# Linear attention, Fourier mixing and two MLPs on one core: the feature projection with each head in its own 64 rows of the array, other banks, folds on GpSimd, other orders at the edges of the MLPs

## The reference

```python
def phi(x):                                   # 128 features, both signs: 256
    proj = einsum('bhsd,df->bhsf', x, w_phi)
    proj = proj - max(abs(proj), axis=-1)
    return concatenate([exp(proj), exp(-proj)])
kv = einsum('bhsf,bhsd->bhfd', phi(k), v);  z = sum(phi(k), axis=2)
x = phi(q) @ kv / (phi(q) @ z + 1e-6)         # attention, heads side by side
u = x + real(fft(fft(x, axis=1), axis=2))     # Fourier mixing
x = u + relu(normalise(u) @ w_ch1) @ w_ch2    # first MLP, 2048 hidden
u = x + (relu(x.T @ w_tok1) @ w_tok2).T       # token MLP, 256 hidden
out = u + relu(u @ w_ch1) @ w_ch2             # second MLP, 1536 hidden
```

## Time and profile before

| | |
|---|---|
| time, median of 3 runs | 996.82 us (995.91 to 997.04) |
| the profiled execution | 994.59 us |
| its span in the trace | 992.8 us |
| TensorE busy | 976.1 us |
| VectorE busy | 379.6 us |
| ScalarE busy | 285.4 us |
| GpSimd busy | 183.5 us |
| TensorE's granted clock | 1.00 of full speed throughout |

### The profile page before, as it was taken

How to read it: one execution, slowest core, us unless ns; L and a number is a source line. 1 busy time by engine, 2 the same in 40 slices (tenths; PEclk the granted TensorE clock), 3 DMA queues, 4 the chain that set the end, 5 groups by cost and what they waited for, 6 DMA issues and landing times.

```text
span 992.8 us, 17316 instructions
## 1 busy us (share of the span) xinstructions
PE 976.1 (98%) x7275; PEld 878.1 (88%) x7275; DVE 379.6 (38%) x756; ACT 285.4 (29%) x573; POOL 183.5 (18%) x161
## 2 busy tenths in 40 slices
PE   8999999999999999999999999999999999999998
PEld 6999999888899999899999999777999999999997
DVE  6998888851422222313213213553121212121211
ACT  6865656533411111111111112343111111111110
POOL 3653556279500000000000000136000000000000
PEclk9999999999999999999999999999999999999999
DMA  7242241426210010010100300775010201001000
GB/s 230 81 109 61 68 135 42 165 96 198 90 64 1 1 64 1 11 53 0 63 0 0 112 1 1 251 279 196 1 64 1 64 1 48 16 32 32 31 1 32
DMA packets 48398, 66.88 MB, mean 67 GB/s; under 512 B 22864, under 2 KB 23888, under 8 KB 48208
## 3 DMA queue, kind: packets, MB, share of 16 engines
q1 hardware_dynamic: 46608, 59.69, 18.5%
q10 hardware_dynamic: 1728, 6.29, 1.7%
HBM read 47.10 MB, written 18.87 MB: 66 GB/s over the span
## 4 chain that ended last, share of the span: by engine, by line
PE 90%; DVE 5%; POOL 2%; ACT 1%; issue 1%; DMA 1%; SPq 0%; DVEq 0%; ACTq 0%; POOLq 0%
PE mlp_y L1060 12%; PE mlp_y L1061 12%; PE mlp_hid L1045 11%; PE mlp_hid L1047 11%; PE mlp_hid L1046 11%; PE mlp_y L1059 11%; PE kv L325 3%; PE num L339 2%; PE proj L296 2%; PE mlp_turn_in L1030 1%; DVE pm L633 1%; DVE absmax L625 1%; PE proj L298 1%; PE proj L297 1%; PE four L350 1%; PE tok_y L1361 1%
## 5 line engine op out<-in xcount | busy, mean ns | idle before, releaser
L1178 DVE SCALAR_TENSOR_TENSOR mlp_h_lo<-mlp_hid,mlp_h_hi 128x384 fp32r<-128x384 f32 x168 | 93.6, 558 | 465.7 <-ACT mlp_h_hi L1095 465.6
L1045 PE MATMUL mlp_hid<-mlp_ut_hi,mlp_w_hi 128*128 128x384 f32 x672 | 229.0, 341 | 0.7 <-POOL mlp_w_lo L1007 0.7
L1095 ACT ACTIVATE mlp_h_hi<-mlp_hid 128x384 fp32r<-128x384 f32 x168 | 82.5, 492 | 501.1 <-PE mlp_hid L1047 500.9
L1047 PE MATMUL mlp_hid<-mlp_ut_hi,mlp_w_lo 128*128 128x384 f32 x672 | 226.5, 337 | 0.0
L1046 PE MATMUL mlp_hid<-mlp_ut_lo,mlp_w_hi 128*128 128x384 f32 x672 | 225.4, 335 | 0.0
L1061 PE MATMUL mlp_y<-mlp_w_hi,mlp_h_lo 128*128 128x512 f32 x504 | 199.4, 396 | 0.0
L1060 PE MATMUL mlp_y<-mlp_w_lo,mlp_h_hi 128*128 128x512 f32 x504 | 198.9, 395 | 0.0
L1059 PE MATMUL mlp_y<-mlp_w_hi,mlp_h_hi 128*128 128x512 f32 x504 | 197.2, 391 | 1.4 <-DVE mlp_h_lo L1178 1.4
L1007 POOL TENSOR_TENSOR mlp_w_lo<-mlp_w_raw,mlp_w_hi 128x1024 fp32r<-128x1024 f32 x26 | 61.7, 2393 | 403.7 <-DVE tok_x_lo L1419 383.3
L1045 PEld LDWEIGHTS mlp_hid<-mlp_ut_hi,mlp_w_hi 128*128 128x128 f32 x672 | 126.3, 188 | 6.5 <-issue 1.1
L1046 PEld LDWEIGHTS mlp_hid<-mlp_ut_lo,mlp_w_hi 128*128 128x128 f32 x672 | 126.3, 188 | 5.3
(11 more groups left out here) (141 smaller groups left out, 1080.8 us busy)
## 6 DMA issues: line engine op xcount, KB each, us to landing
mlp_u<-u_scratch SPq DMA_DIRECT2D x12, 768.0 KB, 4.6
mlp_w_raw<-in_w_mlp SPq DMA_DIRECT2D x14, 512.0 KB, 4.9
mlp_w_raw<-in_w_mlp ACTq DMA_DIRECT2D x12, 512.0 KB, 5.6
v<-in_v SPq DMA_DIRECT2D x16, 320.0 KB, 3.6
qk<-in_kT SPq DMA_DIRECT2D x16, 288.0 KB, 4.1
qk<-in_qT SPq DMA_DIRECT2D x15, 288.0 KB, 4.2
u_scratch<-x_all SPq DMA_DIRECT2D x4, 1024.0 KB, 4.8
x_scratch<-mlp_u SPq DMA_DIRECT2D x5, 768.0 KB, 3.6
```

Source lines behind the costliest of these rows:

```text
L1045: nc.tensor.matmul(out, w_hi[:, j, col], hi, start=(c == 0), stop=False)
L1047: last = nc.tensor.matmul(out, w_lo[:, nf - 1 - j, col], hi, start=False, stop=(c == DC - 1))
L1095: nc.scalar.activation(h_hi[:, j % 2, :], hid[j % 2][:, 0:BT], ACT.Relu).then_inc(h_rounded, 1)
L1178: nc.vector.scalar_tensor_tensor(out=h_lo[:, j % 2, :], in0=hid[j % 2][:, 0:BT], scalar=0.0, in1=h_hi[:, j % 2, :], op0=ALU.max, op1=ALU.s ...
```

## The change

The projection takes each head by itself: 64 rows of the stationary tile of tokens times 128 columns of w_phi in the same rows. The two heads go to two banks, alternately. KA and KB are filled together (one head's keys each), likewise QA and QB, so that there are three fills: REST, KA and QA. A unit is now one head's 512 tokens, and `ek` and the queries' order follow that. In steps without many Fourier pieces (`plain`), fills alternate between `proj` and the two Fourier banks. kv is cut in two parts by head. The steps' lists are written out anew: the norm of the pair before comes directly after REST on VectorE, and in the last step ScalarE and VectorE take the MLP input ahead of the Fourier piece of slot 3. All folds go to GpSimd but for the last pair's, which is on VectorE. In GpSimd's queue the split of keys is made three pairs ahead instead of two, behind the fold, and the last third of a batch and its row come one step later; SyncE stores batch 0 in iteration 13 instead of 11, and batch 1 behind the load of the MLP's first block. In the token MLP's `FIRST` the last three token tiles instead of two are finished for one half before the other. Before the second MLP the rounding of the last four weight chunks is spread.

```diff
-    proj = [bank("proj0"), bank("proj1")]
-    four = [bank("four0"), bank("four1")]
+    proj = bank("proj", 2)
+    four = bank("four", 2)
...
+    def plain(step):
+        return step < 5 or step % 4 < 2
+    def on_four(step, unit):
+        return plain(step) and (unit == KA) == (step % 2 == 1)
+    def banks_of(p, unit):
+        return four if on_four(p.n - 1, unit) else proj
...
-            if n in (11, 15):
-                store(sp, n // 4 - 2)
+            if n == 13:
+                store(sp, 0)
         sp.wait_ge(qk_split, 2 * PAIRS)
         sp.wait_ge(u_stored[0], 32)
         mlp1["load_block"](sp, 0)
+        store(sp, 1)
         sp.wait_ge(u_stored[1], 32)
         mlp1["load_early"](sp)
...
-    def pe_project(pe, p, unit):
+    def pe_fill(pe, p, unit):
...
-        wait_if(pe, shifted, 5 * p.n + unit - 1)
-        out_bank = proj[(p.parity + unit) % 2]
-        for j in range(1 if unit == REST else 2):
+        step = p.n - 1
+        if plain(step) and unit == REST and step >= 8 and step % 4 == 0:
+            for n in range(2):
+                pe_bank_free(pe, step // 4 - 2, len(PIECES) - 1 - n)
+        elif plain(step):
+            wait_if(pe, shifted, 5 * p.n + {REST: -2, KA: 0, QA: 1}[unit])
+        else:
+            wait_if(pe, shifted, 5 * p.n + {REST: 0, KA: 1, QA: 3}[unit])
+        banks = banks_of(p, unit)
+        tiles = 1 if unit == REST else 4
+        for j in range(tiles):
             tokens = slice(FIRST[unit] + 128 * j, FIRST[unit] + 128 * j + 128)
             hi, lo = qk_hi[:, p.parity, tokens], qk_lo[:, p.parity, tokens]
-            out = out_bank[:, 2 * F * j:2 * F * j + 2 * F]
-            nc.tensor.matmul(out, hi, wphi_hi[:, :], start=True, stop=False)
-            nc.tensor.matmul(out, hi, wphi_lo[:, :], start=False, stop=False)
-            last = nc.tensor.matmul(out, lo, wphi_hi[:, :], start=False, stop=True)
-        last.then_inc(proj_done, 1)
+            for n, (x, w) in enumerate(((hi, wphi_hi), (hi, wphi_lo), (lo, wphi_hi))):
+                for h in range(2):
+                    rows = slice(DH * h, DH * h + DH)
+                    col = 512 * h + F * j
+                    last = nc.tensor.matmul(banks[:, col:col + F], x[rows, :], w[rows, F * h:F * h + F],
+                                            start=(n == 0), stop=(n == 2))
+                    if j == tiles - 1 and n == 2 and (h == 1 or unit != REST):
+                        last.then_inc(proj_done, 1)
...
     def pe_step(pe, k):
+        if not last:
+            pe_fill(pe, Pair(following), REST)
+        pe_slot(pe, k, 0)
+        if k >= 0:
+            pe_turn(pe, p, 0)
+            pe_kv(pe, p, 0)
+        pe_slot(pe, k, 1)
+        if not last:
+            pe_fill(pe, Pair(following), KA)
+        pe_slot(pe, k, 2)
+        if k >= 0:
+            pe_turn(pe, p, 1)
+            pe_kv(pe, p, 1)
+            pe_turn(pe, p, 2)
+        if last:
+            mlp1["first_in"]["tensor"](pe, 0)
+            mlp1["first_in"]["tensor"](pe, 1)
+        pe_slot(pe, k, 3)
+        if last:
+            mlp1["first_in"]["tensor"](pe, 2)
+            mlp1["first_in"]["tensor"](pe, 3)
+        else:
+            pe_fill(pe, Pair(following), QA)
+        pe_slot(pe, k, 4)
+        if k >= 0:
+            pe_num(pe, p)
...
+    def dve_last_fold(dve):
+
+        cols = slice(D - 2 * DH, D)
+        dve.wait_ge(x_done, PAIRS)
+        dve.wait_ge(odd_folded, 2 * B - 1)
+        x = x_of(LAST)
+        nc.vector.tensor_tensor(fold_d[:, :, cols], x[:, 0:FRONT, cols], x[:, 5:2:-1, cols],
+                                ALU.subtract).then_inc(last_differed, 1)
         nc.vector.tensor_tensor(fold_s[:, :, cols], x[:, 0:FRONT, cols], x[:, 5:2:-1, cols],
                                 ALU.add).then_inc(summed, 1)
+        low, high = MIRROR[1]
+        dve.wait_ge(summed, PAIRS)
         nc.vector.tensor_tensor(fold_s[:, :, low], fold_s[:, :, low], fold_s[:, :, high],
                                 ALU.add).then_inc(even_folded, 1)
...
+        dve.wait_ge(last_differed, 1)
+        dve.wait_ge(edge_made, 2 * B)
+        nc.vector.tensor_tensor(fold_d[:, :, low], fold_d[:, :, low], fold_d[:, :, high],
+                                ALU.subtract).then_inc(odd_folded, 1)
...
     def dve_step(dve, k):
...
+            dve_shift(dve, following, REST)
+        dve_slot(dve, k, 0)
+        if k >= 1:
+            dve_norm(dve, Pair(k - 1))
+        dve_slot(dve, k, 1)
+        if not last:
+            dve_shift(dve, following, KA)
+        dve_slot(dve, k, 2)
+        if last:
+            mlp1["first_in"]["vector"](dve, 0)
+            mlp1["first_in"]["vector"](dve, 1)
+            dve_slot(dve, k, 3)
...
+        dve_shift(dve, following, KB)
+        if k % 4 == 1 and 5 <= k:
+            dve_low(dve, k // 4 - 1, 0)
+            dve_low(dve, k // 4 - 1, 1)
+        dve_slot(dve, k, 3)
+        dve_shift(dve, following, QA)
+        dve_slot(dve, k, 4)
+        dve_shift(dve, following, QB)
...
     def act_step(act, k):
...
+        if k >= 0:
+            act_qexp(act, p, 1)
+        if last:
+            mlp1["act_weights"](act, [1])
+        if k >= 0:
+            act_kv(act, p)
+            act_qexp(act, p, 2)
+        if folding:
+            act_fold(act, k // 4 - 1, 1)
+        if last:
+            mlp1["first_in"]["scalar"](act, 0)
+            mlp1["first_in"]["scalar"](act, 1)
+            act_slot(act, k, 3)
...
     def pool_step(pool, k):
         b = k // 4 - 1
         if k + 2 < PAIRS:
-            pool_split(pool, Pair(k + 2))
+            pool_split(pool, Pair(k + 2), QUERY)
+        if k % 4 == 2 and b >= 1:
+            pool_add(pool, b - 1, 2)
+            pool_row(pool, b - 1)
+        if k > 0:
+            pool_fold(pool, Pair(k - 1))
+        if k + 3 < PAIRS:
+            pool_split(pool, Pair(k + 3), KEY)
...
-        if k % 4 == 0 and b >= 1:
+        if k % 4 == 1 and b >= 1:
             pool_add(pool, b - 1, 1)
...
-        pool_add(pool, LAST, 0)
         pool.wait_ge(d_done, 2 * FRONT * B)
         mlp1["gpsimd"](pool, (), 4, 6)
+        pool_add(pool, LAST, 0)
...
-    FIRST = [(t, j) for t in range(KT - 2) for j in range(MT)] + [(t, j) for j in range(MT) for t in (KT - 2, KT - 1)]
+    FIRST = [(t, j) for t in range(KT - 3) for j in range(MT)] + [(t, j) for j in range(MT) for t in range(KT - 3, KT)]
...
+                for c in range(DC):
+                    mlp2["first_in"]["scalar"](act, c)
+                    if c:
+                        mlp2["act_weights"](act, [MLP2_CHUNKS[b][c - 1]])
+            def mlp2_last_weight(act, j):
+                if j == 1:
+                    mlp2["act_weights"](act, [NF2 - 1])
```

277 lines of the change are left out of this document (118 added, 159 removed).

## The result

The changed kernel takes 1007.8 us (median of 4 runs, 1006.3 to 1008.9) against 996.6 us before: 1.0117 times the time, 95% interval 1.0104 to 1.013. It is slower; 990.6 us, which is faster, was forecast. The profiled execution has a span of 1005.9 us, 13.1 us more than the 992.8 us of before.

What follows compares the result with a forecast made beforehand. TensorE, busy 98% of the span, was taken as the bound, VectorE near its limit. Terms +0.6 - 2.1 - 1.0 - 0.5 - 1.9 - 1.3 = -6.2 us gave 990.6 us from 996.8; range 978 to 1010.

Steps and rivals of the forecast that it cites:

- The pair: Projection: two row-half matmuls overlap and take 0.115 us a pair, 0.10 us less per step.
- serial loads: Rival: weight loads of the two row halves don't overlap, 3.2 us more a step, about 1041 us; chance 0.17.
- faster pair: Rival: a projection pair takes 0.062 to 0.10 us, giving 968 to 984 us; chance 0.08.
- Breaks: Attention steps: nine changes of kind instead of six breaks add 0.14 us; with projection, 9.56 to 9.60 us, +0.6 over 15.
- The rule that I weighed as a rival: Attention steps: changes of kind cost 0.25 us each when rows are split, 14 us in all, 1005 us; chance 0.11.
- VectorE's delays: Attention steps: VectorE's work falls to 7.9 us a step, so TensorE's delays go, -2.1 us.
- The last attention step: Last attention step: ScalarE's reordering gives back about 2 us, late weights cost 1; net -1 us.
- The other rule: Projection: load time goes by columns, not rows; 54 loads one after another would give 5.8 us a step, about 1033 us.
- early weights: Last attention step: first two MLP weight chunks load about 4 us later; charged 1 us of 0 to 4.
- ScalarE's new order: Last attention step: both MLP input chunks come ahead of the Fourier piece on ScalarE, giving back about 2 us.
- MLP head: Start of first MLP: fold and low-part changes +0.4, a vanished weight-chunk wait -0.9; sum -0.5 us.
- Token MLP and second MLP: Later stages: earlier hidden half saves 1.9 us, spread roundings before the second MLP save 1.3 us.

Runs made afterwards that it cites:

- full_kv_whole: Changed kernel with projection on all 128 rows, kv of both heads together except in the last step, and slot 0's differences first there: 994.83 us.
- full_rows_256: Changed kernel with the projection back to 27 matmuls of 256 columns over all 128 rows, order of fills, queues and folds kept: 1003.41 us.
- kv_whole: Changed kernel with kv matmuls of both heads together behind the second transposes in all attention steps but the last, row-split projection kept: 1004.59 us.
- slot0_first: Changed kernel with VectorE making slot 0's differences before normalizing the MLP's first block in the last attention step: 1005.13 us.
- edges_kv_first: Kernel before with the token MLP and second MLP edits, plus ScalarE's kv copy, last query exponentials and first two roundings ahead of slot 3's copies: 990.46 us.
- edges_alone: Kernel before with only the two later-stage edits, in the token MLP and ahead of the second MLP: 992.77 us.
- warm_18: Changed kernel with 18 instead of 11 warming matmuls at the start: 1008.02 us.
- start_order: Changed kernel with 18 warming matmuls and ScalarE's rounding of pair 2's keys behind the first pair's key exponentials: 1006.9 us.
- odd_on_gpsimd: Changed kernel with the very last odd fold back on GpSimd behind its edge, instead of on VectorE: 1007.04 us.

## Why the prediction was wrong

Between the profiles of before and after the sum has -6.2 us and the measurement +13.1, 19.3 us apart: 9.0 in the 14 steps (-1.5 forecast, +7.5 measured), 5.7 in the last step, 2.4 at the start, 2.0 in the first MLP and 0.2 behind it.

**The pair** was right: 0.115 us taken, 0.111 measured. The serial loads (1041 us) are thus ruled out, and so is the faster pair. The sum behind 0.115 was an estimate from kv pairs and two drawn load times; that it came within 0.004 us doesn't show that it is what sets the pace. The pace gives 27 x (0.119 - 0.111) = 0.21 us a step back.

**Breaks: this is the step that failed.** It said that new changes of kind, "at 0.05 to 0.1 us like those of rows 3, less the wait between two units, add 0.14 us". full_kv_whole has the same fills with four changes in a plain step (num to fill, transposes to kv, kv to transposes, fill to num); the changed kernel has nine, since the transposes and num now border on row halves and kv is cut. So five changes were added, where I added three to my count of six breaks. The two plain steps are apart by 9.87 - 9.39 = 0.48 us, and with the 0.21 that the pairs save that is 0.69 us for five changes, 0.14 us each. Against before (9.56 us) the sum is +0.69 for changes, -0.21 for the pace and -0.17 for three fills instead of five units: the measured +0.31. I had +0.04.

The 0.14 us are a mean. Cutting kv alone costs 0.2 us for each of its two changes when the projection is full work (full_rows_256 against full_kv_whole), and the three changes that row halves add to full_rows_256 cost 9.87 - 9.80 + 0.21 = 0.28 us, 0.09 each.

The cause of the wrong size is in how was read. I took "four transposes take 0.44 us (0.11 each)", which is a mean over a group that ends in a change and one that doesn't, and then counted six breaks to share 0.49 us. (72 num instructions at 0.0311 us are 2.24 us, not 2.27, which changes little.) The timeline of before has both groups. One is in the earlier trace rows, 44.44 to kv at 44.96, 0.52 us; the other is the first row here:
```profile
42.41 0.60 PE L311 MATMUL pt<-mlp_ident,pm 128*128 128x128 f32 x4
42.76 0.36 PE L296 MATMUL proj<-wphi_hi,qk_hi 128*128 128x256 f32 x1
42.96 0.28 PE L297 MATMUL proj<-wphi_lo,qk_hi 128*128 128x256 f32 x1
...
43.44 0.28 PE L298 MATMUL proj<-wphi_hi,qk_lo 128*128 128x256 f32 x1
...
43.84 0.28 PE L297 MATMUL proj<-wphi_lo,qk_hi 128*128 128x256 f32 x1
```
0.35 us up to full work, which is 0.088 a transpose. The price of a change, 0.17 us, was half hidden in the pace. The borders between transposes and projection cost 0.08 us at most before (42.76 to 42.96 is 0.20 where 0.12 is the pace); each became a change. The last two rows show what three fills instead of five units give back: from the last matmul of one unit to the second of the next it is 0.40 us where 0.24 is the pace.

The steps with Fourier pieces were left out of this part of the prediction altogether. They have the fills between full Fourier matmuls, so more of the new borders, and grew by 1.2 us (15.04 to 16.25) and 0.85 us (13.48 to 14.33). Row halves make 0.9 and 0.3 us of that (kv_whole, 16.17 and 13.96, against full_kv_whole, 15.25 and 13.69), the order beside them 0.2 in each (full_kv_whole against before), and the cut kv the rest. Taken together the 14 steps cost +7.5 us where the sum had +0.6.

The rule that I weighed as a rival, that a change of tiling mode drains the engine ("TensorEngine Tiling (Array Packing)", section "Key Properties", of the Trainium skill), agrees with the runs: 0.41 us for a piece of 0.11 us or less between blocks of another mode. This rival had 1005 us and a chance of 0.11. It had the right mechanism, with 0.25 us a change where 0.14 on the mean was measured, and had no cost for the start or the last step; its total came near because these errors cancel, which is luck.

The other rule, that the time of a weight load goes by its columns ("TensorE: Matmul & The Clock Gate", section "LDWEIGHTS (loading the stationary operand)"), doesn't decide here: a load of 128 columns is drawn 190 ns before and 192 to 197 ns on row halves, and yet the pace is 0.111 us a pair, with two loads in it.

**VectorE's delays** (-2.1 us forecast) were mis-sized. The 2.1 us were what the windows left over, and most of it was not waiting for VectorE: 1.8 of the 2.5 us of waits for pm in the earlier trace rows lie before the first num, and in the 14 steps one step is longer by such waits (10.28 us where 9.56 is usual), 0.7 us. These went. The three steps of a Fourier batch take 39.8 us before and 40.2 in full_kv_whole, so nothing was gained there. With the borders taken out, the new order, the gain in plain steps included, is worth 0.85 us over 14 steps (164.03 to 163.18).

**The last attention step** (-1.0 us forecast, +4.7 measured) is the second failure. I followed ScalarE's and GpSimd's queues, charged the early weights, and did not follow VectorE's: the diff moves the normalizing ahead of slot 0's differences, and TensorE's Fourier piece waits for these. slot0_first gave 3.8 of the 4.7 us back, the clock's share included. The gain from ScalarE's new order was real, and edges_kv_first adds it to edges_alone: -1.9 us in the last step (-1.5 against before, whose clock did not fall there), 2.2 us by the two ratios, where I had 2.

**The start** has no term in the sum; it cost 2.4 us in this profile and up to 5.4 in others with the same start. In warm_18 and start_order TensorE, with fills of four tiles, ran ahead of VectorE, its idle time came in one piece of 1.58 and 1.53 us, and the clock was 0.50 behind it. In the changed kernel itself the clock is 0.50 from 9 us on with no wait since 7.0, and why is not shown.

**MLP head** (-0.5 us forecast, +1.5 measured): the mechanism, that the first low part of the hidden layer "is now queued behind the edge and the odd fold", is what happened, 1.67 us of wait instead of the 1 us forecast, and odd_on_gpsimd takes back 1.4 us. The wait for a weight chunk at 228.64 went as forecast, but 0.43 us of wait for one stands at 260.42 instead, and the wait of 1.08 us at 268.04 had no term. What makes this last one was not tried.

**Token MLP and second MLP** (-3.2 us forecast) were right: -3.0 measured, and -3.3 by the medians of edges_alone.

## What to carry to other kernels

On an engine with tiled modes, price the border before the block: here a change between full, row-half and column-half work cost 0.14 us on the mean, 0.09 to 0.2 by kind, where one matmul of 256 columns takes 0.119 us. A split that saves 0.008 us on each of 27 pairs, 0.21 us, pays for one or two such borders, and this change added five. To read that price from a trace, find two groups of the same work that end in different neighbours, and compare starts; a mean over both hides it. When a diff rewrites a step's order for several engines, follow each of the queues through the first and the last step as well, where nothing is in its steady state, and test the edits apart: the useful part of this change, 5.4 us by the ratio of edges_kv_first, was three small edits outside the projection.
